# Attention in front of a feed-forward and an expert stage: pairs of heads in four steps, tile 0's scores in fp32, reciprocals spread through memory

## The reference

```python
B, H, S, D = 4, 8, 576, 64
scores = q @ k.transpose(0, 1, 3, 2) / sqrt(D)
scores = where(block_i >= block_j, scores, -1e9)      # blocks of 64 positions
scores = scores - max(scores, axis=-1)
attn = exp(scores)
attn = attn / (sum(attn, axis=-1) + 1e-09)
x = (attn @ v), heads side by side: [B * S, H * D]
x = elu(x @ w_in) @ w_out
x = routed experts of x (gate, w1, relu, w2)
```

## Time and profile before

| what | value |
|---|---|
| median of 3 runs | 852.62 us (850.96 to 853.86) |
| the profiled execution | 851.58 us, span 849.9 us |
| mean granted TensorE clock in it | 0.987 |
| PE busy | 814.4 us, 96% of the span, 4730 instructions |
| DVE busy | 532.2 us, 63% |
| ACT busy | 360.8 us, 42% |
| POOL busy | 240.9 us, 28% |

### The profile page before, as it was taken

The page is one execution under the profiler, slowest core; times in us unless marked ns, Lnnn a source line. Parts: engine busy times, 40 slices in busy tenths (PEclk is TensorE's granted clock), DMA queues, the critical chain, the costliest instruction groups (busy, mean ns, idle before and its releaser), DMA issues.

```text
span 849.9 us, 15007 instructions
## 1 busy us (share of the span) xinstructions
PE 814.4 (96%) x4730; PEld 673.6 (79%) x4731; DVE 532.2 (63%) x1306; ACT 360.8 (42%) x879; POOL 240.9 (28%) x232
## 2 busy tenths in 40 slices
PE   5999999998799999999999999999997999999995
PEld 4777777775698998898898888889885777887884
DVE  4766676776433378658758748843755799376342
ACT  4766766764233322232232232232443487165141
POOL 3656655662344112002101102100102233122121
PEclk9999999999799999999999999999999999999998
DMA  6344444521423222021020020050241599364000
GB/s 151 96 110 122 123 110 114 152 81 55 142 61 132 86 78 71 1 84 29 1 85 19 10 75 1 25 198 1 100 156 42 198 298 368 118 200 161 31 26 8
DMA packets 97505, 83.30 MB, mean 98 GB/s; under 512 B 63460, under 2 KB 74980, under 8 KB 97328
## 3 DMA queue, kind: packets, MB, share of 16 engines
q1 hardware_dynamic: 94400, 77.68, 29.6%
q0 software_dynamic: 3056, 5.00, 1.8%
HBM read 67.54 MB, written 18.27 MB: 101 GB/s over the span
## 4 chain that ended last, share of the span: by engine, by line
PE 69%; DVE 2%; issue 1%; DVEq 1%; ACT 0%; POOL 0%; POOLq 0%; ACTq 0%
PE h_ps L1557 11%; PE out_ps L1557 11%; PE h_ps L1558 11%; PE h_ps L1559 11%; PE out_ps L1559 11%; PE out_ps L1558 11%; PE out_ps L1692 1%; PE tr_ps L1657 1%; PE lg_ps L1608 1%; DVEq L858 0%; DVE xt_lo L1265 0%; PE tr_ps L1597 0%; DVE ht_lo L1304 0%; DVE x2t L1294 0%; DVE tile_ids L1274 0%
## 5 line engine op out<-in xcount | busy, mean ns | idle before, releaser
L1395 ACT ACTIVATE ex<-h_ps 128x384 f32<-128x384 f32 x96 | 47.3, 492 | 277.6 <-PE h_ps L1559 277.6
L1557 PE MATMUL h_ps<-xt_hi,wi_hi 128*128 128x384 f32 x384 | 133.1, 347 | 5.3 <-DVE xt_lo L1265 5.3
L1558 PE MATMUL h_ps<-xt_lo,wi_hi 128*128 128x384 f32 x384 | 131.0, 341 | 0.0
L1559 PE MATMUL h_ps<-xt_hi,wi_lo 128*128 128x384 f32 x384 | 131.0, 341 | 0.0
L1233 DVE TENSOR_SCALAR ex<-ex 128x384 f32<-128x384 f32 x96 | 35.0, 365 | 145.2 <-ACT ex L1395 144.0
L1557 PE MATMUL out_ps<-wo_hi,gt 128*128 128x512 f32 x288 | 114.6, 398 | 0.0
L1559 PE MATMUL out_ps<-wo_hi,gt 128*128 128x512 f32 x288 | 113.9, 396 | 0.0
L1558 PE MATMUL out_ps<-wo_lo,gt 128*128 128x512 f32 x288 | 113.3, 393 | 0.0
L425 ACT ACTIVATE prob<-s_ps,negmax 128x128 f32<-128x128 f32 (+2 forms) x144 | 78.0, 549 | 13.7 <-DVE negmax L305 7.2
L1115 DVE CUSTOM_DVE_ANT_0 x2t<-x,w_raw 128x512 bf16<-128x512 f32 x108 | 82.7, 806 | 0.4
L1557 PEld LDWEIGHTS h_ps<-xt_hi,wi_hi 128*128 128x128 f32 x384 | 73.1, 190 | 9.3 <-DVE xt_lo L1265 6.0
(11 more groups left out here) (177 smaller groups left out, 1690.0 us busy)
## 6 DMA issues: line engine op xcount, KB each, us to landing
w_raw<-in_moe_w_dram SPq DMA_DIRECT2D x56, 512.0 KB, 5.2
attn_t<-attn_sb SPq DMA_DIRECT2D x16, 288.0 KB, 2.2
x_raw<-attn_t SPq DMA_DIRECT2D x24, 192.0 KB, 2.5
out_dram<-x SPq DMA_DIRECT2D x18, 256.0 KB, 2.3
x_rows<-x SPq DMA_DIRECT2D x18, 256.0 KB, 2.6
raw_qk<-in_q_dram SPq DMA_DIRECT2D x32, 128.0 KB, 2.4
raw_qk<-in_k_dram SPq DMA_DIRECT2D x32, 128.0 KB, 2.5
v<-in_v_dram SPq DMA_DIRECT2D x32, 128.0 KB, 2.4
```

The source lines that it names most:

```text
L1395: act.activation(ex[:, f % 2], h_ps[:, f % 2, 0:NB], ACT.Exp).then_inc(ex_done, 1)
L1557: pe.matmul(dst, stat[0], mov[0], start=start, stop=False, skip_group_check=True)
L1558: pe.matmul(dst, stat[0], mov[1], start=False, stop=False, skip_group_check=True)
L1559: return pe.matmul(dst, stat[1], mov[0], start=False, stop=stop, skip_group_check=True)
```

## The change

- A pair is one step on every engine (`all_pairs`) with one order for each. Tiles 0 and 1 are scored one after the other into the same two banks of s_ps (columns 0 and 128), tile 2 and LAST into the other two, tile 3 into the first again. VectorE's maxima of tiles 0 and 1 wait for both, and so do ScalarE's exponentials.
- Tile 0's scores are one fp32 product for each head, from qk_f, in place of three passes. The wait for the split stays.
- The tails of q and k are loaded into one tile (`raw_tail`, q in rows 0 to 63, k in 64 to 127) and turned at once. That turn goes to bank 1 of t_ps, after tile 1's turns; ScalarE copies it after tile 3's exponentials.
- The nine columns of recip are turned at once, beside tile 0's turns of the next pair; VectorE copies the 9 x 128 result to r_rows; SP stores it to memory (`store_recips`) and loads it back by four broadcasting DMAs into r_sb (`load_recips`). `spread_recips`, `recip_rows`, `turn_recips` are gone. The columns of negmax, rowsum and recip are sorted by head.
- The values run in two parts.
- SP's order in a step: load v, store of the older pair, store of the past pair's reciprocals, load q and k, load of the reciprocals, load w_in.

GpSimd's code is the same. The diff, cut to its core:

```diff
-    PARTS = [PIECES[0:2], PIECES[2:4], PIECES[4:]]
+    PARTS = [PIECES[0:4], PIECES[4:]]
+    R0 = BANK - P
...
+        def s_pair(u):
+            bank, col = {0: (0, 0), 1: (0, P), 2: (2, 0), 3: (0, 0)}[u]
...
+        def s_last():
+            return s_ps[:, 2 * BANK + S4:2 * BANK + S4 + S]
...
             def load_qk(n, i):
                 wait(sp, prep_t, 3 * (n - 1))
-                load(q, n, raw[i][:, 0], qk_in[i])
-                load(k, n, raw[i][:, 1], qk_in[i])
+                load(q, n, raw[i][:, 0], raw_tail[i][0:TAIL], qk_in[i])
+                load(k, n, raw[i][:, 1], raw_tail[i][TAIL:P], qk_in[i])
...
+            def store_recips(n):
+                wait(sp, r_row_done, n + 1)
+                sp.dma_start(r_dram, r_rows[:, :]).then_inc(r_stored, 16)
+
+            def load_recips(n):
+                wait(sp, r_stored, 16 * n + 16)
+                for h in range(2):
+                    rows = slice(h * D, (h + 1) * D)
+                    sp.dma_start(r_sb[rows, 0:FULL * P], r_dram[h * FULL:(h + 1) * FULL, :]
+                                 .rearrange("(o u) q -> o (u q)", o=1).broadcast_to([D, FULL * P]))\
+                      .then_inc(r_in, 16)
+                    sp.dma_start(r_sb[rows, FULL * P:S], r_dram[COLS - 1:COLS, rows]
+                                 .broadcast_to([D, TAIL])).then_inc(r_in, 16)
...
-                if (past := pair(kk, i, -2)):
-                    store(*past)
+                if (older := pair(kk, i, -2)):
+                    store(*older)
+                if (past := pair(kk, i, -1)):
+                    store_recips(past[0])
                 if (ahead := pair(kk, i, 3)):
                     load_qk(*ahead)
+                if past:
+                    load_recips(past[0])
...
             def turned_corner(n, i, last):
...
+                wait(dve, r_stored, 16 * n)
+                dve.tensor_copy(r_rows[:, :], t_ps[0:COLS, 1, R0:R0 + P]).then_inc(r_row_done, 1)
...
             def final(n, i):
                 wait(dve, pv_done, n + 1)
-                wait(dve, r_out, 2 * n + 2)
+                wait(dve, r_in, 64 * n + 64)
...
+            def step(kk, i):
+                now, past, older = pair(kk, i), pair(kk, i, -1), pair(kk, i, -2)
+                if now:
+                    row_max(now[0], 0)
+                    row_max(now[0], 1)
+                if past:
+                    for h in range(2):
+                        turned_head(*past, 3, h)
+                if older:
+                    final(*older)
+                if past:
+                    recips(past[0])
+                    turned_last(*past)
+                if now:
+                    row_max(now[0], 2)
+                if past:
+                    turned_corner(*past, last=not now)
+                if now:
+                    turned_pair(*now, 0)
+                    row_max(now[0], 3)
+                    turned_pair(*now, 1)
+                    row_max(now[0], LAST)
+                    for h in range(2):
+                        turned_head(*now, 2, h)
...
+                if now:
+                    exp(*now, 0)
+                    exp(*now, 1)
+                    if after:
+                        prep_copy(*after, 0, 0)
+                        prep_copy(*after, 1, 0)
+                    exp(*now, 2)
+                    exp(*now, 3)
+                    if after:
+                        prep_copy(*after, 2, 1)
+                    exp(*now, LAST)
+                    guard(*now)
...
             def scores(n, i, u):
-                wait(pe, exp_done, exps(n, u - 2, 1) if u >= 2 else exps(n - 1, u + 3, 1))
                 if u == 0:
+                    wait(pe, exp_done, exps(n - 1, 3, 1))
                     wait(pe, split_lo, 2 * n + 2)
+                elif u > 1:
+                    wait(pe, exp_done, exps(n - 1, LAST, 0) if u == 2 else exps(n, u - 2, 1))
...
+                if u == 0:
                     for h in range(2):
+                        pe.matmul(dst[:, h], qk_f[i][rows[h], mine], qk_f[i][rows[h], K:K + w],
+                                  start=True, stop=True, skip_group_check=True)
...
+            def step(kk, i):
+                now, past, older, after = pair(kk, i), pair(kk, i, -1), pair(kk, i, -2), pair(kk, i, 1)
+                if now:
+                    scores(*now, 0)
+                    scores(*now, 1)
+                if past:
+                    for h in range(2):
+                        turn_head(past[0], 3, h)
+                if older:
+                    values(*older, 1)
+                if after:
+                    wait(pe, turned, turns(past[0], 3, 0)) if past else pe.wait_ge(prep_out, 3)
+                    prep(*after, 0, 0)
+                if past:
+                    turn_last(past[0])
+                if now:
+                    scores(*now, 2)
+                    if after:
+                        wait(pe, prep_out, 3 * after[0] + 1)
+                        prep(*after, 1, 0)
+                    turn_pair(now[0], 0, past=past)
+                    scores(*now, 3)
+                    turn_pair(now[0], 1, after)
+                    if after:
+                        wait(pe, turned, turns(now[0], 0))
+                        prep(*after, 2, 1)
+                    scores(*now, LAST)
+                if past:
+                    if not now:
+                        turn_corner(past[0])
+                    values(*past, 0)
+                if now:
+                    for h in range(2):
+                        turn_head(now[0], 2, h, after)
```

More of the change, by code:

```diff
@@ L183, in _, with load @@
         def _(sp):
-            def load(t, n, dst, landed):
+            def load(t, n, dst, tail, landed):
                 heads = t.rearrange("b h s d -> (b h) s d")[bass.ds(2 * n, 2)]
@@ L241, in _ @@
                     step(kk, i)
-            for i in range(2):
-                store(PAIRS - 2 + i, i)
+            store(PAIRS - 2, 0)
+            store_recips(PAIRS - 1)
+            load_recips(PAIRS - 1)
+            store(PAIRS - 1, 1)
             for i in range(2):
@@ L520, in turn_pair, with turn_head @@
                         last = turn(bank, (h * c + j) * P, prob[u][h][:, j * P:(j + 1) * P])
-                if u == 0 and not (isinstance(n, int) and n == 0):
-                    last = turn(bank, 2 * P, prob4[:, FULL * P:S])
+                if u == 0 and past:
+                    turn(bank, 2 * P, prob4[:, FULL * P:S])
+                    last = turn(bank, R0, recip[:, :])
                 last.then_inc(pt_done, 1)
-            def turn_head(n, u, h):
+            def turn_head(n, u, h, ahead=None):
                 wait(pe, exp_done, exps(n, u, h))
@@ L529, in turn_head @@
                     wait(pe, turned, turns(n, 2, h))
[L530 to L534 removed]
+                elif h == 0:
+                    wait(pe, turned, turns(n, 1))
+                elif ahead:
+                    wait(pe, prep_out, 3 * ahead[0] + 3)
                 else:
[L536 removed]
+                    wait(pe, turned, turns(n, 0))
                 for j in range(u + 1):
@@ L550, in turn_corner @@
                 wait(pe, turned, turns(n, LAST))
-                turn(1, 2 * P, prob4[:, FULL * P:S]).then_inc(pt_done, 1)
-            def turn_recips(n, ahead, alone):
-                wait(pe, spread, n + 1)
-                if ahead:
-                    wait(pe, prep_out, 3 * (n + 2) + 3)
-                else:
-                    wait(pe, turned, turns(n, 3, 0))
-                for u in range(FULL):
-                    last = turn(0, u * P, recip_d[:, 2 * u:2 * u + 2, :].rearrange("p h d -> p (h d)"))
-                last.then_inc(r_turned, 1)
-                wait(pe, turned, turns(n + 1, 0 if alone else 1))
-                turn(1, 0, recip[:, COLS - 1:COLS].to_broadcast([P, P])).then_inc(r_turned, 1)
+                wait(pe, rec_done, n + 1)
+                turn(1, 2 * P, prob4[:, FULL * P:S])
+                turn(1, R0, recip[:, :]).then_inc(pt_done, 1)
             def values(n, i, part):
@@ L584, in _, with step @@
                 prep(0, 0, g, (0, 1, 0)[g])
-            def step(kk, i, u):
+            def step(kk, i):
                 now, past, older, after = pair(kk, i), pair(kk, i, -1), pair(kk, i, -2), pair(kk, i, 1)
                 if now:
-                    scores(*now, u)
-                if u == 0:
-                    if past:
-                        for h in range(2):
-                            turn_head(past[0], 3, h)
-                    if older:
-                        values(*older, 2)
-                    if now and after:
-                        wait(pe, turned, turns(past[0], 3, 0)) if past else pe.wait_ge(prep_out, 3)
-                        prep(*after, 0, 0)
-                if u == 1:
-                    if past:
-                        turn_last(past[0])
-                    if now and after:
+                    scores(*now, 0)
[13 more added lines that the diff above has]
```

(15 more changed lines are left out.)

155 lines of the change are left out of this document (51 added, 104 removed).

## The result

The changed kernel takes 883.62 us in the median of 4 runs (879.17 to 884.34), the one before, run beside it, 851.79 (849.70 to 853.86). The ratio is 1.0363, 95% interval [1.0319, 1.0406]: slower by 32 us. The profiled execution took 883.70 us with a span of 882.0; the span before was 849.9.

What follows compares the result with a forecast made beforehand. TensorE's issue bounds pairs at 12.40 us; the change would make a 13.75 us loop the bound. 851.58 profiled plus 25.4 (18.9 loop, 3.8 first pair, 2.7 end) plus 3.1 clock gives 880.1, median 881, range 862 to 904.

Steps and rivals of the forecast that it cites:

- a loop through the split: Attention pairs: scores, tile 3's exponentials, tail copies, GpSimd's split, next scores; 13.75 us, 1.35 more a pair, 18.9 in all.
- the clock: New 2.4 us TensorE waits lower its clock at a pair's head; two falls of 1.55 us taken, 3.1 us.
- the first pair: Attention stage's first pair grows from 9.54 to 13.4 us by the same loop: 3.8 more, bounds 3.4 and 4.2.
- the end: Last pair's scaling waits for reciprocals sent through memory: 2.7 us later, bounds 1 and 5.
- TensorE's own work: What TensorE must issue per attention pair: falls by 1.06 us to 11.34 us.
- The fp32 term: Tile 0's scores on TensorE: two fp32 passes, 0.25 us, replace three passes, 0.33 us; saves 0.08 us.
- The other terms: TensorE savings per pair: reciprocals' turns 0.42 us, q and k tails 0.10, fewer changes between turns and products 0.3, wait 0.16.
- Its four stretches: Tile 0's to tile 3's scores 6.05 us; through tile 3's exponentials 3.73; tail copy to split 0.77; split to TensorE 3.20.
- The rival with a fall in most pairs: TensorE's clock falls in most pairs, 1.55 us each, 23 us in 15 pairs: 900 us; chance 0.16.
- The cover in the middle pairs: Reciprocals' trip through memory ends 1.6 us into the next pair, scaling waits until some 3.2; costed at nothing.
- The rival "faster": The loop through GpSimd's split does not hold and TensorE's 11.34 us a pair decide: 838 us; chance 0.07.
- The signs named ahead: Profile: 13.7 us pairs, 2.4 us qk_lo waits, split after tail copies, last scaling released by r_sb's DMA, single clock dips.

Runs made afterwards that it cites:

- number 10: number 9 with tile 0's scores put back from one fp32 product to three fp32r passes: 837.01 us, ratio 0.9834.
- number 1: Changed kernel with ScalarE copying the q and k tails ahead of tile 3's exponentials, not after them: 855.90 us, ratio 1.0052.
- number 4: Changed kernel with eighteen needless TensorE turns of the identity after tile 2's turns, filling its wait: 872.09 us, ratio 1.0243.
- number 3: Changed kernel with SyncE loading the reciprocals back ahead of the q and k loads: 882.13 us, ratio 1.0370.
- number 2: Changed kernel with GpSimd's split in three parts (q, k, tails), tile 0's scores waiting for the first two only: 855.09 us, ratio 1.0043.
- number 9: Changed kernel with number 2's split and another SyncE order: store pair, store reciprocals, load v, load reciprocals, then q and k: 836.45 us, ratio 0.9823.
- number 7: Changed kernel with the edits of number 1, number 2 and number 3 together: 851.37 us, ratio 1.0000.
- number 12: number 9 with the next stage's four x_raw loads on SyncE moved behind the last pairs' steps: 836.52 us, ratio 0.9821.

## Why the prediction was right, and where it was off

The forecast, 881 us and a loop through the split, came true: 883.6, inside the range of 862 to 904. The mechanism was right; that the sum came within 3 us is in part luck, for its misses offset one another: the clock and the first pair cost 7.9 and 1.6 us more than I had summed, the loop, the end and the rest of the kernel, which I had put at nothing, 2.4, 1.6 and 1.8 less. Step by step:

- **TensorE's own work:** 11.34 us predicted, 11.08 measured. The fp32 term, 0.08, was measured by number 10. The other terms were not taken apart.
- **The loop:** 13.75 predicted, 13.53 measured. Its four stretches: 6.05 and 5.90, 3.73 and 3.72, 0.77 and 0.75, 3.20 and 3.16. Fourteen starts cost 16.5 us instead of 18.9. That the loop is the cause, numbers 1 and 4 show: opening it gives 28 us back, filling the wait 11.5.
- **The clock:** the mis-sized term. I took two falls, 3.1 us, because the new waits are just shorter than that of the earlier trace rows. There were six, in four of which the low level lasted 3.4 us and in two 6.8, and 11.0 us. The rival with a fall in most pairs had the price right for a turn with a short fall (1.5 to 1.6 us in three of the four; the long ones cost 2.9), but six turns in a row had none. The waits ahead of turns with a fall and of turns without one are alike, 2.4 to 2.7 us, so what decides on a fall stays open.
- **The first pair:** 3.8 predicted, 5.4 measured. I took tile 0 to tile 3 from a trace in which TensorE had reached its high rate by tile 3; in the changed kernel's profiled execution it reached it later. The stretch took 6.56 us, and ScalarE was free 4.37 after tile 3's scores instead of 3.73. The change does not force this: in numbers 3 and 4 the same work had the high rate at tile 3, and the first pair took 13.55 and 13.56 us, against 13.4 forecast. So 1.4 us of the 5.4 differ from one execution to another; what decides them no run shows.
- **The end:** 2.7 predicted, 1.1 measured. From the corner copy's end to the scaling 5.98 us passed where I had 6.63. I priced the store's landing by the gates' trip, 2.43 us; the load was issued 1.2 us after the store (242.36 to 243.59). The four issues were as predicted, and the last landing took some 0.5 more. The other 1.0 I had not counted: from the last pair's scores to the corner copy's end 15.8 us passed instead of 16.8.
- **The cover in the middle pairs:** costed at nothing, rightly, but with 1.6 us to spare. The last load was issued at 113.66, and by the median of these loads, 2.6 us, it had landed at about 116.3, against a scaling at 117.06: some 0.7. I wrote that as slack, where it was the next bound: with the split's loop open the pair stopped at 12.5, not at TensorE's 11.1 (numbers 1, 2). The rival "faster", 838 us, is what numbers 9 and 10 reach, and it took a split in three and another order on SyncE.

The signs named ahead held: 13.53 us a pair, 2.45 us of wait for qk_lo, the split right behind the tail copies, dips of the clock, no wait for r_sb in the middle pairs. One did not: the profile puts the last scaling's wait down to "issue", not to a DMA.

## What to carry over

When a change reorders the work of several engines, follow each loop from one turn to the same point of the next through every engine, and price the second-longest as well as the longest: here the split stood at 13.53 and the trip of the reciprocals near 12.5, over 11.08 of work, and moving the loads right behind their store made SyncE's own row a third bound at some 12.3. A copy that another engine's preparation waits for goes ahead of that engine's own long instruction, and a wait for a store's landing is covered by issuing something else in between. A short recurring wait on TensorE can cost through the clock too: here 11.0 us, beside the 16.5 of the longer loop.

## What was not expected of the hardware

- Filling a wait with needless turns made the kernel 11.5 us faster (number 4).
- SyncE's issuing can be a bound: 16 issues, 0.3 to 0.7 us each, with one wait of 1.4 took 12.4 us of a pair (number 7). The Trainium skill, DMA: Bandwidth & Descriptors, Issuing engines are not separate DMA queues, calls the time to initiate a DMA usually small against the DMA; here a broadcasting load took 0.60 us to issue and 2.6 to land, and the issues in a row, not the transfers, set the pace.
- A small store could be read back soon, but not always: 1.2 us after its issue the load behind it went out at the end of the changed kernel, 1.8 in number 7, and over 4.5 in one pair each of numbers 9 and 12.
